# One change to an attention and two-layer feed-forward kernel: both quads' merged matrices as 64x32 products, and loads of k, q, v over 128 partitions

## The reference, cut to what matters

```python
packed = softmax(scale * p @ k.T) @ v            # per batch and head: 32 x 64
out    = softmax(scale * q @ packed.T) @ packed  # 576 x 64
x      = out as (B*S, H*D) = (4608, 512)
h      = x @ w_in                                # 4608 x 1024
...    # softmax times h, layer norm, @ w_out -> 512 features
y      = max(x2 @ w1, x2 @ w2, x2 @ w3) @ w_out2 # 4608 x 512
```

## Time and profile before

| what | value |
|---|---|
| median of 3 runs | 1096.2 us (1093.41 to 1096.96) |
| the profiled execution | 1094.8 us, span of its instructions 1093.2 us |
| PE / DVE / ACT / POOL busy | 94% / 55% / 32% / 23% of the span |
| attention stage, 0 to 190 us | DMA share 0.89, 213 GB/s, PE busy 141.6 us |
| granted TensorE clock, mean | 0.978 |

### The profile page before, as it was taken

The page is one execution under the profiler, slowest core; times in us unless marked ns, Lnnn a source line. Parts: engine busy times, 40 slices in busy tenths (PEclk is TensorE's granted clock), DMA queues, the critical chain, the costliest instruction groups (busy, mean ns, idle before and its releaser), DMA issues.

```text
span 1093.2 us, 15814 instructions
## 1 busy us (share of the span) xinstructions
PE 1030.2 (94%) x6498; PEld 815.8 (75%) x6498; DVE 606.3 (55%) x980; ACT 345.6 (32%) x551; POOL 250.8 (23%) x222
## 2 busy tenths in 40 slices
PE   5778868799999999999999999999999999999998
PEld 4444534487888888888888888888888888888887
DVE  1367757767657747765646653667355563654021
ACT  3345544333423414432422233222322142222111
POOL 0112354448398439832000000000000000000000
PEclk9789989899999999999999999999999999999999
DMA  9988985234366145511575444554455535543251
GB/s 201 247 214 205 250 216 148 100 138 156 118 233 227 65 156 179 223 44 77 212 279 188 176 166 162 183 179 179 154 186 176 185 137 191 177 156 112 98 171 39
DMA packets 47144, 183.23 MB, mean 168 GB/s; under 512 B 8032, under 2 KB 8032, under 8 KB 37472
## 3 DMA queue, kind: packets, MB, share of 16 engines
q1 hardware_dynamic: 40848, 147.21, 42.6%
q0 software_dynamic: 6224, 35.00, 8.7%
HBM read 134.62 MB, written 47.58 MB: 167 GB/s over the span
## 4 chain that ended last, share of the span: by engine, by line
PE 78%; DVE 9%; DMA 5%; issue 4%; ACT 2%; POOL 1%; SPq 1%; ACTq 0%
PE ps L1088 27%; PE ps L723 24%; PE ps L1120 13%; PE ps L1111 4%; PE ps L737 2%; PE ps L988 2%; DMA q_raw<-in_q_dram 2%; PE ps L870 2%; DMA w_in_s<-in_moe_w_in_dram 2%; DVE a2T L1570 1%; DMA k_raw<-in_k_dram 1%; DVE h_lo L1479 1%; DVE spot L1776 1%; PE ps L828 1%; DVE spot L1767 1%
## 5 line engine op out<-in xcount | busy, mean ns | idle before, releaser
L1088 PE MATMUL ps<-ys,slot 128*128 128x512 f32 x1512 | 345.8, 390 | 0.5
L1088 PEld LDWEIGHTS ps<-ys,slot 128*128 128x128 f32 x1512 | 283.3, 188 | 62.4 <-ACT spot L1163 3.9
L1767 DVE TENSOR_TENSOR spot<-ps,spot 128x512 f32<-128x512 f32 x108 | 74.3, 688 | 99.7 <-PE ps L1088 74.2
L1163 ACT ACTIVATE spot<-ps 128x512 f32<-128x512 f32 x90 | 52.8, 596 | 207.5 <-PE ps L1088 196.4
L723 PE MATMUL ps<-ln_hi,w_out_s_lo 128*128 128x512 f32 x280 | 109.1, 390 | 0.0
L723 PE MATMUL ps<-ln_hi,w_out_s_hi 128*128 128x512 f32 x280 | 109.0, 389 | 0.0
L723 PE MATMUL ps<-ln_lo,w_out_s_hi 128*128 128x512 f32 x280 | 109.0, 389 | 0.0
L1120 PE MATMUL ps<-w_out_s_lo,h_hi 128*128 128x512 f32 x216 | 84.1, 389 | 0.0
L1120 PE MATMUL ps<-w_out_s_hi,h_lo 128*128 128x512 f32 x216 | 84.1, 389 | 0.0
L1120 PE MATMUL ps<-w_out_s_hi,h_hi 128*128 128x512 f32 x216 | 84.1, 389 | 0.0
L1294 ACT ACTIVATE u<-ps,neg_max 128x1024 f32<-128x1024 f32 x36 | 40.2, 1117 | 124.0 <-DVE neg_max L1645 124.0
(11 more groups left out here) (152 smaller groups left out, 1500.9 us busy)
## 6 DMA issues: line engine op xcount, KB each, us to landing
slot<-w_operands SPq DMA_DIRECT2D x36, 1792.0 KB, 7.3
w_operands<-stage POOLq DMA_DIRECT2D x18, 1024.0 KB, 4.9
k_raw<-in_k_dram SPq DMA_DIRECT2D x32, 288.0 KB, 5.9
v_raw<-in_v_dram SPq DMA_DIRECT2D x16, 576.0 KB, 9.4
q_raw<-in_q_dram SPq DMA_DIRECT2D x16, 576.0 KB
y_features<-yst SPq DMA_DIRECT2D x9, 1024.0 KB, 4.4
y_raw<-y_features SPq DMA_DIRECT2D x9, 1024.0 KB, 5.6
out_dram<-spot SPq DMA_DIRECT2D x36, 256.0 KB, 2.1
```

What stands on the lines that cost most here:

```text
L1088: last = pe.matmul(ps[:, group_bank(g, k), :], w[:, a - 1, i, kk, :], ys[:, b, j, kk, :], start=n < 4 and kk == 0 and e == 0, stop=kk == K ...
L1163: return act.activation(dst, src, ACT.Copy)
L1767: dve.tensor_tensor(dst[:, :], a, b, op).then_inc(ready, 1)
```

## The change

Three things. (1) Loads of k, q and v go head by head: one DMA for each h takes that head of both quads and writes all 128 partitions; the HBM side of it is now described as [2 quads][64 partitions][576 numbers] where it was [64 partitions][heads][576 numbers]. k stays at four DMAs a batch, q and v go from two to four. (2) `w_in` is laid out as the heads by quad ([half g] x h instead of pairs of heads) and loaded by four DMAs of 512 KB, their HBM side described as [2 quads][64 rows][1024 numbers], instead of one of 2048 KB. (3) `merge(b)` makes both quads together, 16 matmuls of 64 rows x 32 columns with 512 columns of `w_in_s`, without the zero blocks, in place of two calls of four matmuls of 128 x 64. It stands where `merge(b, 1)` stood, behind `turn_packed`, in steps 0 to 5, and at the end of step 6; `copy_m(6, 1)` on ACT moves to the end of step 6 as well.

```diff
-    w_in_v = w_in.rearrange("(k p) n -> p k n", p=P)
+    w_in_v = w_in.rearrange("(g h d) n -> h g d n", g=QUADS, d=D)
     def rows(t):
-        return t.rearrange("b (g h) (p j) d -> b g p h (j d)", g=QUADS, j=J)
+        return t.rearrange("b (g h) (p j) d -> b h g p (j d)", g=QUADS, j=J)
             def load_k(b):
                 if b > 0:
                     sp.wait_ge(kT_filled, (QH + 1) * b)
-                for x in range(2):
-                    for g in range(QUADS):
-                        sp.dma_start(k_raw[half(g), 2 * x:2 * x + 2, :, :].rearrange("p h j d -> p h (j d)"),
-                                     k_v[b, g][:, 2 * x:2 * x + 2, :]).then_inc(k_loaded[x], 16)
+                for h in range(QH):
+                    sp.dma_start(k_raw[:, h, :, :].rearrange("p j d -> p (j d)"), k_v[b, h]).then_inc(k_loaded[h // 2], 16)
             def load_v(b):
-                for g in range(QUADS):
-                    sp.dma_start(v_raw[half(g), :, :, :].rearrange("p h j d -> p h (j d)"), v_v[b, g])\
-                        .then_inc(v_loaded, 16)
+                for h in range(QH):
+                    sp.dma_start(v_raw[:, h, :, :].rearrange("p j d -> p (j d)"), v_v[b, h]).then_inc(v_loaded, 16)
...
                 if b == 0:
-                    sp.dma_start(w_in_s[:, :, :], w_in_v).then_inc(w_in_loaded, 16)
+                    for h in range(QH):
+                        sp.dma_start(w_in_s[:, h, :], w_in_v[h]).then_inc(w_in_loaded, 16)
...
-            def merge(b, g):
-                bank = wide_banks[g]
+            def merge(b):
                 pe.wait_ge(*turn_done("packed", b))
                 if b == 0:
-                    pe.wait_ge(w_in_loaded, 16)
+                    pe.wait_ge(w_in_loaded, 16 * QH)
                 if b == B - 1:
-                    pe.wait_ge(m_copied[g], B - 1)
-                elif g == 1:
+                    for g in range(QUADS):
+                        pe.wait_ge(m_copied[g], B - 1)
+                else:
                     pe.wait_ge(packed_first, b + 2)
                     pe.wait_ge(packed_second, b + 2)
-                elif b == B - 2:
-                    pe.wait_ge(h_used, 1)
+                    if b == B - 2:
+                        pe.wait_ge(h_used, 1)
                 for n in range(2):
-                    for l in range(2):
-                        last = pe.matmul(ps[l * 2 * NPACK:(l + 1) * 2 * NPACK, bank + n, :], pair_of(packedT[b % 2], 2 * g + l),
-                                         w_in_s[:, 2 * g + l, n * 512:(n + 1) * 512], start=True, stop=True)
-                last.then_inc(m_filled[g], 1)
+                    for h in range(QH):
+                        for g in range(QUADS):
+                            last = pe.matmul(ps[h * NPACK:(h + 1) * NPACK, wide_banks[g] + n, :],
+                                             packedT[b % 2][half(g), QH * g + h, 1 - g, :],
+                                             w_in_s[half(g), h, n * 512:(n + 1) * 512], start=True, stop=True)
+                            if n == 1 and h == QH - 1:
+                                last.then_inc(m_filled[g], 1)
```

More of the change, by code:

```diff
@@ L302, in token_of @@
         return J - 1 if m == 0 else 2 * ((m - 1) % STEPS) + (m - 1) // STEPS
-    def pair_of(t, pair):
-        return t[:, 2 * pair:2 * pair + 2, :, :].rearrange("c h t n -> c (h t n)")[:, NPACK:3 * NPACK]
     def main_cols(t, part, h, g):
@@ L439, in load_q @@
                     sp.wait_ge(qT_filled, (QH + 1) * b)
-                for g in range(QUADS):
-                    sp.dma_start(q_raw[half(g), :, :, :].rearrange("p h j d -> p h (j d)"), q_v[b, g])\
-                        .then_inc(q_loaded, 16)
+                for h in range(QH):
+                    sp.dma_start(q_raw[:, h, :, :].rearrange("p j d -> p (j d)"), q_v[b, h]).then_inc(q_loaded, 16)
             def load_in(b):
@@ L815, in turn_q @@
                 if j == 0:
-                    pe.wait_ge(q_loaded, 32 * b + 32)
+                    pe.wait_ge(q_loaded, 64 * b + 64)
                 turn_rows(bank, q_raw, j).then_inc(qT_filled, 1)
             def pack(b):
-                pe.wait_ge(v_loaded, 32 * b + 32)
+                pe.wait_ge(v_loaded, 64 * b + 64)
                 pe.wait_ge(a1T_first, 2 * b + 2)
@@ L942, in step @@
                     turn_q(b + 1, 0)
-                if third and first:
-                    merge(b, 0)
                 if second:
@@ L947, in step @@
                     turn_packed(b + 1)
-                if third:
-                    merge(b, 1)
+                if third and first:
+                    merge(b)
                 if second:
@@ L1275, in step @@
                     copy_m(b, 0)
+                    copy_m(b, 1)
             act.wait_ge(zeroed, 4)
```

## The result

The changed kernel takes 1531.53 us (median of 4 runs, 1531.13 to 1532.01) against 1096.26 us before: ratio 1.398, 95% interval 1.3952 to 1.4003. The prediction was 1555 us, 1500 to 1650. The profiled execution took 1531.87 us, its span is 1530.1 us.

What follows compares the result with a forecast made beforehand. DMA nearly full in the first 190 us, PE after. Last q at 578 + 41 + 26 + 3 = 648 us instead of 185.6: 1094.8 + 462 - 3 for the merge = 1554, or 1555 us on the runs' scale; range 1500 to 1650.

Steps and rivals of the forecast that it cites:

- What bounds the kernel: First 190 us: DMA engines busy 0.89 at 213 GB/s, so the sum hangs on when the last q lands.
- How many engines: Changed loads: outermost HBM count of 2 puts each DMA on two engines instead of sixteen; two at full rate given 0.81.
- the width sets an engine's rate: Loads: 64 partitions give 13.2 to 14.1 GB/s an engine, 128 should give about 24.5.
- k, q and v: Their loads, 28.3 MB on two engines at 49 GB/s, take 578 us.
- w_in: Its load, 2.10 MB at 51.5 GB/s in the same queue between q(1) and k(3), takes 41 us.
- The rest, with start and landing: Before the last q: the two engines' share of p, w_out and stores 26 us, first issue and last landing 3 us.
- the queue doesn't run dry: SP's load queue: the next q is issued long before it empties, 0 us; up to 40 us kept for the high end.
- The low end of the bounds: Whole kernel, all loads at 25.8 GB/s an engine: 549 + 41 + 25 + 3 = 618 us, total 1523 us.
- Behind the last q: After the last q: an otherwise unchanged tail of about 906 us, with 3 us saved by the shorter merge.
- Sixteen engines: Rival, chance 0.13: all sixteen engines share each load, stage bound by PE and handing over; -35 us, 1060 us.
- Engines at half rate: Rival, chance 0.02: two engines, each no faster than 13.2 to 14.1 GB/s; total about 2000 us.
- products of different quads in series: Rival, chance 0.02, with sixteen engines: the merge's 16 products run one after another, 13.6 us a batch; about 1130 us.

Runs made afterwards that it cites:

- 62 and 2 cut: Kernel before, every load of k, q, v cut in two by partitions, 62 and 2 of each 64, same plain pattern: 1503.74 us.
- 124 and 4 cut: Kernel with even and odd quads, every load of k, q, v cut by partitions into 124 and 4: 1239.66 us.
- even and odd quads: Changed kernel with quads made of even and odd heads, k, q, v loads fused to 128 partitions, w_in in one DMA: 1071.67 us, ratio 0.9764.
- apart edit: Kernel with even and odd quads, in step 6 the merge of quad 1 and its copy back in their earlier places: 1071.60 us, ratio 0.9767.
- loads alone: Kernel before with only the change's loads of k, q, v; w_in and the merge as before: 1494.18 us.

## Why the prediction was right, point by point

**What bounds the kernel, and the question that follows from it.** Right: the time moved by 435 us and the last q by 435.4 us.

**How many engines.** This was the step taken at 0.81 from the form of the counts and the rule of the Trainium skill, with no row of before to show it. It holds: share 0.13, 52 GB/s, two packets in flight. The 62 and 2 cut shows that the number's divisors do it, the 124 and 4 cut that the rate goes with them. The step before it, that the width sets an engine's rate, was right for sixteen engines only: two of them did 26.2 GB/s each on 62 partitions.

**The terms of the sum.** k, q and v: 578 us forecast. 96 issues at 5.6 us make 538 us, since an engine did 26.3 GB/s and not the 24.5 taken between w_out's 23.9 and w_in's 25.8. Both of these were sixteenths of a full set; two engines by themselves reached slightly more than either. w_in: 41 us forecast, 40 by its bytes at 52.5 GB/s. The rest, with start and landing: 29 us forecast; 621 - 538 - 40 = 43 us were left. It is not the volume, for the changed kernel moved 40.48 MB up to 621 us and 40.5 were forecast; what the 14 us are was not measured. That the queue doesn't run dry was right for two engines. Together: the last q at 621 us instead of 648, a miss of 27 us in which the rate is -40 and the rest +14. That two misses of opposite sign cancel in part is luck; without the second the forecast would have been some 40 us off, still inside its range.

The low end of the bounds adds up to 1524 us, not 1523, which changes nothing.

**Behind the last q.** Forecast 906.2 us of the execution's own time, measured 910.9. Here the 3 us to be saved were not. The merge itself is nearly as fast as forecast, two quads in 1.96 us at full clock (638.99 us) against 3.65, where 1.7 had been worked out. (All eight products of the scores end within 0.69 us, not 0.61: the row with twelve records is six of them.) But the forecast took its 3 us from the 3.63 us of L870 in the chain, and misread them. They were one quad only, and at the halved clock. Before, its clock in a window, and then POOL's timeline behind it:

```profile
195.26:198.89 3.63, 3.63 (x17) 0.79 (x21) 1.72 (x6) 0.59 (x1) 0.00 (x0) 0.50 0.36 144
```

```profile
200.25 0.55 POOL L662 DMA_DIRECT2D m_merged<-merged  x1 [5.72 <-ACT merged L1163]
...
206.01 2.27 POOL L646 TENSOR_TENSOR a<-a,m 128x576 f32<-128x576 f32 x2
```

In the changed kernel both quads of step 6 stand in that place, at the halved clock again, and the chain holds 3.66 us of them: nothing is saved. Both copies now follow, and POOL's store, the last split of w_out and the subtraction for the last batch stand in line behind them: the subtraction comes 22.1 us after the last q is taken up, 20.4 before. The shorter `merge(7)` is not on the chain. With even and odd quads the apart edit takes back 1.4 us in the profile, though not in the time. It shows one thing more: a quad by itself takes 1.92 us at full clock as 64x32 products too, as it did with 128x64 (1.94). The gain comes from the two quads side by side, not from the smaller shape:

```profile
162.06 1.92 PE L865 MATMUL ps<-w_in_s,packedT 64*32 64x512 f32 x16
```

Five executions have tails of 906.0 (loads alone), 909.0 (62 and 2), 909.2 (before), 910.4 (124 and 4) and 910.9 us (changed), so of the 4.7 us between forecast and measurement a few may be scatter.

**The rivals.** Sixteen engines was priced at 1060 us (1045 to 1085) and came out at 1071.67 us when built with even and odd quads. Of the 51 us that loads had on the chain, 17.4 us are left there (k 10.7, q 6.7 us), so 33 us went, as priced (35). But the last q moved by only 22 us: the rest was picked up by what stands next in line. One piece of that is `up(0, 0)`, which at half clock takes 5.49 us ahead of the last q in this execution; the others were not measured apart. Engines at half rate and products of different quads in series are both excluded, by 26.3 GB/s an engine and by 1.96 us for 16 products.

## What to carry to other kernels

Count what the outermost dimension of both sides of a DMA is after all fusing; if the two have no large common divisor up to 16, the load runs on few engines, and neither its width in SBUF nor its bytes help. With k engines the signs are a DMA share near k/16 and SP issues as long as the transfer. A better layout of the loads is often a matter of which index is paired with which: even and odd heads gave 128 fused partitions and 2.4% where quads of neighbours gave a loss of 40%.

## What was not expected of the hardware

TensorE's clock was granted at half, 1.2 GHz, in long stretches in which PE did little. In the changed kernel it was 0.56 from 120 to 150 us, with PE busy 6.94 of 30 us, and 0.50, full half, from 150 to 200 us, with PE busy 2.46 of 50 us (the windows above). In the kernel before, the stage ran at 0.90 with PE busy 141.6 of 190 us. So transposes of q took 1.94 us for eight records where they took 1.07.

The window of 0 to 60 us reads 1.00, with PE busy 7.65 us, but this is not a granted clock. The changed kernel's trace holds no clock record before 78.9 us, and the view shows 1.00 where there is none. The transposes tell the clock there:

```profile
15.35 1.94 PE L731 MATMUL ps<-ident,k_raw 128*128 128x128 f32 x8 [15.35 <-DMA k_raw<-in_k_dram]
```

They are as slow as at 0.50. Up to the last q this cost nothing, since PE was waiting for loads; behind it the first transposes took 0.9 us more than before. What lets the clock rise again was not tested.
